# Attention, then two mixtures of experts, on one core: a piece of the products with the values stands ahead of a tile's transposes instead of behind them

## What is computed

```python
# q, k, v: (2, 8, 768, 64); proj: (64, 6)
q_bucket = sum(((q @ proj) > 0) * powers)      # 6 bits for each row, k_bucket likewise
mask     = q_bucket[:, :, :, None] == k_bucket[:, :, None, :]
scores   = where(mask, q @ k.T / 8, -1e9)
attn     = exp(scores - max(scores)); attn = attn / (sum(attn) + 1e-9)
x        = (attn @ v) as 1536 rows of 512
x        = moe(x)       # each row to one of 8 experts, 192 rows each, taken greedily by gate score
out      = moe2(x)      # rows with x @ w_skip > 0 go to their best expert, the others stay
```

## Time and profile before

| | us |
|---|---|
| median of 3 runs | 630.75 (629.92 to 631.79) |
| the profiled execution, its own time | 632.04 |
| its span | 630.0 |

### The profile page before, as it was taken

One profiled execution on the slowest core, in us unless ns is written; L12 is line 12 of the kernel. 1 busy time (PEld: TensorE's weight loads), 2 busy tenths in 40 slices (PEclk: granted clock), 3 DMA queues, 4 the chain that ended last, 5 costly groups with the idle time before them and its releaser, 6 DMA issues.

```text
span 630.0 us, 11469 instructions
## 1 busy us (share of the span) xinstructions
PE 607.7 (96%) x4384; PEld 474.2 (75%) x4384; DVE 360.2 (57%) x1132; ACT 292.7 (46%) x525; POOL 147.3 (23%) x153
## 2 busy tenths in 40 slices
PE   7899999999999999888999999999999889999997
PEld 4667777767766765478898989899999867777774
DVE  5877776776776777787787878696502220000000
ACT  4877787777777678243534525251212201111111
POOL 6440303132133904101010101011333123333201
PEclk8999999999999999999999999999999999999999
DMA  7938936546473100644343627364896869999970
GB/s 176 239 84 187 216 90 152 126 110 162 106 217 67 32 4 2 232 161 160 134 166 128 227 85 269 121 230 150 269 324 242 303 214 335 351 344 352 332 271 20
DMA packets 73393, 116.38 MB, mean 185 GB/s; under 512 B 33799, under 2 KB 37161, under 8 KB 73058
## 3 DMA queue, kind: packets, MB, share of 16 engines
q1 hardware_dynamic: 68738, 106.75, 55.2%
q0 software_dynamic: 4016, 8.80, 4.0%
q10 hardware_dynamic: 576, 0.01, 0.0%
HBM read 87.76 MB, written 12.23 MB: 159 GB/s over the span
## 4 chain that ended last, share of the span: by engine, by line
PE 83%; DVE 6%; DMA 6%; issue 2%; ACT 2%; POOL 0%; SPq 0%; POOLq 0%; DVEq 0%
PE psB L1070 13%; PE psB L1084 11%; PE psB L356 10%; PE psB L1816 8%; PE psB L1831 8%; PE psA L326 6%; PE psB L341 6%; PE psA L328 5%; DMA xg<-x_scratch,recs 2%; PE psB L371 2%; DVE mx L477 2%; PE psA L1006 2%; DMA x_scratch<-x 1%; PE psB L1107 1%; PE psB L284 1%
## 5 line engine op out<-in xcount | busy, mean ns | idle before, releaser
L477 DVE TENSOR_REDUCE mx<-psA 128x1 f32<-128x768 f32 x96 | 91.6, 954 | 43.9 <-PE psA L328 43.1
L545 ACT ACTIVATE prob<-psA,ebi,esc 128x768 f32<-128x768 f32 x96 | 95.3, 992 | 31.9 <-DVE ebi L422 31.5
L1070 PE MATMUL psB<-xgT,w 128*128 128x192 f32 x512 | 91.9, 332 | 0.3 <-ACT xgT L1170 0.3
L1084 PE MATMUL psB<-hT,w 128*128 128x192 f32 x512 | 88.2, 330 | 0.0
L1070 PEld LDWEIGHTS psB<-xgT,w 128*128 128x128 f32 x512 | 82.5, 190 | 7.4 <-issue 3.6
L1084 PEld LDWEIGHTS psB<-hT,w 128*128 128x128 f32 x512 | 82.7, 190 | 0.3
L326 PE MATMUL psA<-kH,qT 128*128 128x384 f32 x192 | 73.8, 385 | 3.6 <-ACT prob L545 2.2
L1907 DVE SCALAR_TENSOR_TENSOR ob<-psB,recs,xg 128x512 f32<-128x512 f32 (+1 forms) x9 | 6.5, 721 | 108.7 <-PE psB L1831 101.3
L356 PE MATMUL psB<-pT,v_in 128*64 128x384 f32 x360 | 68.0, 499 | 0.0
L341 PE MATMUL psB<-identity_words,prob_words 128*128 128x128 f32 x576 | 64.4, 249 | 0.8 <-DVE pT L490 0.4
L328 PE MATMUL psA<-kB,qB 128*128 128x384 f32 x192 | 64.8, 337 | 0.0
(11 more groups left out here) (290 smaller groups left out, 849.7 us busy)
## 6 DMA issues: line engine op xcount, KB each, us to landing
w<-in_moe_w SPq DMA_DIRECT2D x34, 2048.0 KB, 9.7
kH<-hi SPq DMA_DIRECT2D x30, 192.0 KB
q_in<-in_q SPq DMA_DIRECT2D x16, 192.0 KB, 4.2
k_in<-in_k SPq DMA_DIRECT2D x16, 192.0 KB, 4.3
v_in<-in_v SPq DMA_DIRECT2D x8, 384.0 KB, 3.9
x_scratch<-x_of_batch SPq DMA_DIRECT2D x2, 1536.0 KB, 6.9
x_scratch<-x SPq DMA_DIRECT2D x8, 384.0 KB, 10.7
qT<-hi SPq DMA_DIRECT2D x15, 192.0 KB
```

The costliest lines, as they stand in the source:

```text
L477: nc.vector.tensor_reduce(mx[:, u:u + 1], psS[u % 2][:, :, 0:HALF], AX.XY, ALU.max).then_inc(s_dv, 1)
L545: nc.scalar.activation(prob[:, u % 2, :, :], psS[u % 2][:, :, 0:HALF], ACT.Exp, bias=ebi[:, u:u + 1], scale=esc[:, u:u + 1], accum_out=den ...
L1070: ins = nc.tensor.matmul(ps[:, (f % 2) * CAP:(f % 2 + 1) * CAP], w1[:, k % 2, d, f * P:(f + 1) * P], xgT[:, k % 2, d, :], start=d == 0, st ...
L1084: ins = nc.tensor.matmul(ps[:, (d % 2) * CAP:(d % 2 + 1) * CAP], w2[:, k % 2, f, d * P:(d + 1) * P], hT[:, k % 2, f, :], start=f == 0, sto ...
```

## The change

In groups 1 to 14, at odd n, the step PV(G-1, n // 2) is put into the list ahead of T(u) instead of behind it. In group 0 there is no PV, and group 15 keeps its order.

```diff
@@ -85,6 +85,8 @@
         if G < NGRP - 1 and n in (2, 4) and todo and todo[0][2] < 4:
 
             steps.append(todo.pop(0))
+        if 0 < G < NGRP - 1 and n % 2:
+            steps.append(("PV", G - 1, n // 2))
         steps.append(("T", u))
 
 
@@ -94,8 +96,6 @@
             if n == per - 1:
                 steps.pop()
             continue
-        if G and n % 2:
-            steps.append(("PV", G - 1, n // 2))
         if G > 1 and n == 0:
             steps.append(("X", G - 2))
         elif G == ROWS_AT and n and n % 2 == 0:
```

## The result

The changed kernel takes 637.64 us (median of 4, 636.8 to 639.92), the kernel before beside it 630.42 (629.92 to 631.79). The ratio is 1.0102 with a 95% interval of 1.0073 to 1.013: slower by about 1%, 7.2 us between the medians. The profiled execution took 636.82 us with a span of 634.8.

What follows compares the result with a forecast made beforehand. TensorE was taken to bound the kernel (83% of the chain). Each group goes from 13.74 to 14.23 us; 12 x 0.49 = 5.9 us over the profiled 632.04, 1.3 less for the median: 636.7, range 632.4 to 640.0.

Steps and rivals of the forecast that it cites:

- Effect 1: On TensorE, a tile's transposes no longer wait for DVE's copy of the tile before; 4.5 us of waits go.
- the rival without a late exp: The transposes' wait goes and no stall replaces it: 2.8 us less, 627.9; chance 0.09.
- Effect 2: TensorE's work per pair without waits: value products start 0.27 us after the last score matmul starts; group sum 13.61 us.
- the rival without the pause: Array need not empty between scores and value products: each pair 0.10 us shorter, total 633.0; chance 0.14.
- Effect 3: Exp starts 1.23 us behind the moved transposes by ACT or DVE, next scores 1.13 later: at least 2.36 us.
- A: First pair of a six-tile group, from its second tile's transposes: stalls on the late exp, forecast 4.67 us.
- B: Second pair, from the group's fourth tile's transposes: stalls on the late exp, forecast 4.72 us against 4.43 now.
- C: Third pair, from the sixth tile, with the next group's first transposes and result projection: no stall, forecast 4.84 us.
- the bits in pair C stand behind T instead of PV: the same work: Making bits (L295) after transposes instead of value products was claimed to add no work; bits cost 0.78 us.
- 12 of 14 groups: Of 14 changed groups 12 were counted as paying 0.49 us each, since some exps are late already: 5.9 us.
- I cost it at nothing: ACT's copy of the value products' result, now ahead of the transposes' copy in pair C: claimed cost nothing.
- The signs asked for: B about 4.7 us, 25 to 28 score waits for exp, no transpose waits for DVE, first value pieces 14.2 apart without bits.

Runs made afterwards that it cites:

- the kernel with DVE's copies: Changed kernel, but behind moved transposes of pairs A and B DVE does scale and bias first, then both copies, ACT none; ratio to before 0.9957.
- the kernel with scale first: Changed kernel with DVE's scale and bias for the exp ahead of its copy of the moved transposes; ratio to before 1.0092.
- the longer and the shorter way: Longer: small ACT copy before exps, changed kernel 1.0152, kernel before 1.0002; shorter: changed kernel, scale first, ACT copying one of four blocks, 199.7 us across the stretch.

## Why the prediction was right

The forecast was 636.7 in a range of 632.4 to 640.0, and 637.64 came; against before, 5.9 us were forecast and 7.2 came, 6.8 of them in the stretch.

- *Effect 1, the wait of T goes*: right. Its price in the rival without a late exp, 2.8 us less, was too high. The kernel with DVE's copies got 0.43% in the total (2.7 us, the interval 1.0 to 4.5), but only 1.2 from X to X: a group with bits came out 0.07 longer and not 0.13 shorter, and one without prep 0.46 shorter and not 0.64.
- *Effect 2, S to PV takes 0.27*: 0.26 measured (123.77 to 124.03); the rival without the pause had 0.17. The Trainium skill (TensorEngine Tiling, Key Properties) says that changing the tiling mode drains TensorE, and the trace agrees as far as it goes: the pause is there at this switch from 128x128 to 128x64 too. What the array does in it no row shows. The pair's 4.41 without waits is 4.42 in the kernel where DVE makes both copies.
- *Effect 3, 1.23 to the exp by both ways, 1.13 to S*: 1.24 and 1.14, by ACT. DVE's way was read too long: its first leg is 0.41 and not 0.47, so 1.17. It did not matter, since ACT's is the longer. That ACT's way sets the exp and S is shown by the kernel with scale first and by the longer and the shorter way.
- *The pairs*: A 4.67 forecast, B 4.72 and C 4.84. Measured A 4.70 (118.43 to 123.13) and B 4.72 (123.13 to 127.85). C without bits is 4.84 (113.59 to 118.43), as forecast; with bits it is 5.76 (127.85 to 133.61), which is 4.98 and not 4.84 besides the 0.78 of the bits.
- *The term that was mis-sized* is this C with bits, "the bits in pair C stand behind T instead of PV: the same work". It is not the same: T and L295 are of different size, so there is one more switch of size in the pair, four where there were three. From T to L295 go 0.65 (130.19 to 130.84 below) where T to S was forecast with 0.54, and S behind L295 is 0.80 long and not 0.77. 0.14 in each of the five groups with bits from X to X is 0.7 us, most of the 0.9 by which the stretch exceeds the forecast of 5.9.

```profile
130.19 0.72 PE L341 MATMUL psB<-identity_words,prob_words 128*128 128x128 f32 x6
...
130.84 0.85 PE L295 MATMUL psB<-raw,pblk 128*32 128x384 f32 x8
...
131.63 0.44 PE L326 MATMUL psA<-kH,qT 128*128 128x384 f32 x1
...
132.43 0.63 PE L341 MATMUL psB<-identity_words,prob_words 128*128 128x128 f32 x6
```

- *12 of 14 groups*: about right. Three groups paid in part: group 12 cost 0.19 (by X 14.27 in place of 14.08) and group 1 0.22 (S to S), since X waited there before, and group 11 0.42, where one S waited for its exp already in the kernel before. The other eleven paid 0.46 to 0.53 without bits and 0.65 to 0.67 with them.
- *"I cost it at nothing" for L606*: right. It runs from 130.31 to 130.79 in pair C, and T's copy, which ACT makes next, waits for TensorE until 130.95. What I had not seen is that the copy's new place is needed: its old one would have cost 9 us more.

The signs asked for came: pair B at 4.72, 24 waits of S (25 to 28 forecast) of 7.5 us beside 2.0 on the matmuls' own row, no wait of T for DVE, PV 0.26 behind the last matmul of S, groups of 14.24 without bits. The group with bits, 15.18, is where the sum was short.

## What to carry to other kernels

A wait that the profile shows is not the only thing that fixes an order: before moving work ahead of an instruction, follow what hangs behind that instruction on the other engines and set its slack, measured from starts, against the length of what is moved. Here 0.70 us of slack stood against a slip of 0.94, and the difference came back as a stall in each pair where TensorE had too little else to do. Where the slack is enough (pair C) or is made so (the copy given to an engine with time), the same move gains; and the stretch that the change touches, measured between two instructions on the bound engine, tells changes of 1 us that totals with 2 us of scatter do not.

## What the runs showed that I had not expected

- A small ACT operation between two others moves the next one by 0.09 us, although it is recorded with 0.19.
- The longer way on ACT cost the order before 0.7 us from X to X although S, in pair B, had 0.7 us of slack behind its exp. Its groups without bits take some 0.1 longer (starts of X 13.84 apart where they were 13.75) and those with bits none. The timeline says where: exp and L606's copy behind it are 0.1 later, and X follows that copy, 0.60 behind T where it was 0.50 (114.47 to 114.97) in the kernel before:

```profile
114.59 0.63 PE L342 MATMUL psB<-identity_words,prob_words 128*128 128x128 f32 x6
...
115.19 0.97 PE L372 MATMUL psB<-pw,xun 128*128 128x144 f32 x6
```

- DVE copies four blocks of 128 in 0.69 us and ACT in 0.59, so that giving the copy to DVE made it 0.10 longer and the kernel faster.
